# Attention scores of the first batch as whole fp32 matmuls over 64 rows, with the activation table loaded early

## The chip, the cores and the metric

The kernel runs on one core of a Trainium2 chip. The metric is the device time of one execution in microseconds. Before the change it was 1102.54 us, the median of three runs (1102.28 to 1103.45 us). All data is fp32.

## The reference

Three layers follow each other on 4 batches x 448 positions = 1792 tokens of width 768:

```python
scores = scale * np.matmul(q, k.transpose(0, 1, 3, 2))     # q, k, v: (4, 12, 448, 64)
scores = cap * np.tanh(scores / cap)
attn = np.exp(scores - np.max(scores, axis=-1, keepdims=True))
attn = attn / (np.sum(attn, axis=-1, keepdims=True) + 1e-09)
x = np.matmul(attn, v)                                     # heads side by side: (1792, 768)
h = np.maximum(np.maximum(x @ w1, x @ w2), x @ w3) @ w_out # 768 -> 768 -> 768
g = h @ w_gate                                             # 768 -> 1536
out = (g * (1 / (1 + np.exp(-g))) * (h @ w_val)) @ w_out2  # 1536 -> 768
```

## The kernel before

**Batches and units.** The dense layers of a batch are 60 units (`UNITS`); a unit is 18 float32r matmuls of 448 columns (L340) against one 128 x 768 block of weights. TensorE runs the units of batch 0, 1, 2, 3 in order. The attention of batch t+1 is spread over the units of batch t: for each of its 6 pairs of heads (`PAIRS`) the tables `SCORE_AT`, `WEIGH_AT`, `VALUE_AT`, `PREP_AT` name the unit that each part stands ahead of. Pair 6 is the first pair of batch 1, and its first scores, `scores(24)`, stand ahead of unit 0 in TensorE's program.

**The first batch's attention** has no dense work beside it. It is a phase of its own, of `FIRST` = 24 steps, four for each pair. A step `a` covers 2 x 112 keys: TensorE makes the scores (`scores`, L265, four float32r matmuls) into `score_ps` or, for odd steps, into two banks of `moe_ps`; ScalarE applies tanh (L395) and exp (L398) into `prob`; TensorE multiplies by v (`values_whole`, L279, two whole fp32 calls, four records). Half of the columns of `v_one` are ones, so that the same matmuls give the softmax sums. After a pair ScalarE copies the sums out (`take_sums`, L405), and VectorE takes the reciprocal (L502), multiplies (L505) and splits the result into `x_hi` and `x_lo` (`split_x`, L514 and L463). TensorE's order is scores(0), scores(1), then scores(a+2), values_whole(a) for each a; scores(a) waits for the tanh of step a-2. In this phase ScalarE also rounds the weights of the first four units (`weights_hi`, L386), one for each of the pairs 1 to 4.

**q and k.** `load_qk(g)` brings a pair's q and k, both heads, twice: into partitions 0 to 63 and again into 64 to 127 of one of the two halves of `qk_raw`. `prepare_qk(g, h)` on VectorE casts one head to `qk_hi` (L470), makes `q_lo` (L463) and subtracts in place for k (L463). The scores matmul thus has 128 rows: k high on the lower 64 and k low on the upper 64, against q in both.

**Queues.** Each engine works through its program in the order written. SyncE issues all loads in order: the qk and v loads of the first batch, then, unit by unit, `load_qk`, `load_v`, `store_lo` and `load_stage`; each has a wait ahead of it, and what stands behind waits with it. VectorE's order in the first phase is `prepare_qk(g + 1, 0)`, `normalise(g - 1)`, `split_x(0, g - 1)`, `prepare_qk(g + 1, 1)` for each g, and last `normalise(5)`, `split_x(0, 5)`. TensorE's units 0 to 2 leave the last chunk of x (pair 5) to the end of unit 2.

Of the kernel before, what the change touches and what calls it, by code (L numbers as in the profile page):

```python
# [9 lines left out]
ACT = mybir.ActivationFunctionType  # L10
ALU = mybir.AluOpType

P = 128
BATCH, HEADS, SEQ, HEAD_DIM = 4, 12, 448, 64
# [3 lines left out]
PAIRS = HEADS // 2  # L18
KEYS = 112
CH = SEQ // KEYS  # L20
HALF = CH // 2
# [13 lines left out]
JOBS = 54  # L35
NP = 4
NQ = 3

FIRST = 4 * PAIRS  # L40
# [31 lines left out]
def build(nc, w_in, qk_in, v_in, cap_in, out):  # L72
    ctx = ExitStack()
    with ctx:
        def sb(name, shape, dt=F32):
            return ctx.enter_context(nc.sbuf_tensor(name, shape, dt))
# [20 lines left out]
        qk_raw = sb("qk_raw", [P, 2, 4, SEQ])  # L97
# [10 lines left out]
        cap = sb("cap", [P, 1])  # L108
        inv_cap = sb("inv_cap", [P, 1])
        tanh_scale = sb("tanh_scale", [P, 1])  # L110

        moe_ps = ctx.enter_context(nc.psum_tensor("moe_ps", [P, BANKS, 512], F32))
        score_ps = ctx.enter_context(nc.psum_tensor("score_ps", [P, HALF, 512], F32))
# [47 lines left out]
        def score_banks(a):  # L161
            return moe_ps[:, 0:HALF, :] if a < FIRST and a % 2 else score_ps

        def value_banks(g):
            return moe_ps[:, 2:4, :] if g < PAIRS and g % 2 == 0 else pv_ps
# [3 lines left out]
        @block.sync  # L169
        def _(sp):  # L170
            def load_stage(u):
                if u >= UNITS + STAGE:
                    sp.wait_ge(w_hi_done, u - STAGE + 1)
                elif u >= STAGE:
                    sp.wait_ge(w_lo_done, u - STAGE + 1)
                sp.dma_start(stage[:, u % STAGE, :],
                             w_in[u % UNITS, :, :]).then_inc(w_loaded[u % STAGE], 16)

            def store_lo(u):
                sp.wait_ge(w_lo_done, u + 1)  # L180
                sp.dma_start(lo_store[u, :, :],
                             w_lo[:, u % R_LO, :].bitcast(F32)).then_inc(lo_stored[u % R_LO], 16)

            def load_lo(u):
                k = u % UNITS
                sp.wait_ge(unit_done, u - R_LO + 1)
                if u < UNITS + R_LO:
                    sp.wait_ge(lo_stored[u % R_LO], 16 * (UNITS // R_LO))
                sp.dma_start(w_lo[:, u % R_LO, :].bitcast(F32),  # L189
                             lo_store[k, :, :]).then_inc(lo_loaded[u % R_LO], 16)  # L190

            def load_qk(g):
                if g >= 2:
                    sp.wait_ge(qk_split, 2 * (g - 1))
                for r in range(2):
                    sp.dma_start(qk_raw[r * HEAD_DIM:(r + 1) * HEAD_DIM, g % 2, :, :],
                                 qk_in[g, :, :, :]).then_inc(qk_loaded[g % 2], 16)

            def load_v(g):
                if g < 2:  # L200
                    sp.wait_ge(ones_done, 4)
                elif g < PAIRS + 2:
                    sp.wait_ge(value_done, 4 * (g - 1))
                else:
                    sp.wait_ge(v_split, g - 1 - PAIRS)
                for h in range(2):
                    sp.dma_start(v_one[:, g % 2, h, :, v_cols[h]],
                                 v_in[g, :, h, :, :]).then_inc(v_loaded[g % 2], 16)

            sp.dma_start(cap[:, :], cap_in).then_inc(cap_loaded, 16)  # L210
            load_qk(0)
            load_v(0)
            load_qk(1)
            load_v(1)
            for u in range(STAGE):
                load_stage(u)
            for g in range(PAIRS):
                load_qk(g + 2)
                if g + 2 <= PAIRS:
                    load_v(g + 2)  # L220
            for u in range(LAST):
                t, k = divmod(u, UNITS)
                g, j = pair_of(t, k)
                if g is not None and j == 0 and PAIRS + 2 <= g + 2 < BATCH * PAIRS:
                    load_qk(g + 2)
                if g is not None and j == 2 and g + 1 < BATCH * PAIRS:
                    load_v(g + 1)
                if t == 0:
                    store_lo(u)
                if u + STAGE < LAST:  # L230
                    load_stage(u + STAGE)
                if UNITS <= u + R_LO < LAST:
                    load_lo(u + R_LO)
# [18 lines left out]

        @block.tensor
        def _(pe):
            def scores(a):
                g, h, c = a // 4, a // 2 % 2, a % 2
                pe.wait_ge(qk_split, 2 * g + h + 1)
                if a >= FIRST:
                    pe.wait_ge(tanh_done, a)
                elif a >= 2:  # L260
                    pe.wait_ge(tanh_done, a - 1)
                for i in range(HALF):
                    k0 = (HALF * c + i) * KEYS
                    for n, q in enumerate((qk_hi[:, h, :], q_lo[:, h, :])):
                        last = nc.tensor.matmul(score_banks(a)[0:KEYS, i, 0:SEQ],  # L265
                                                qk_hi[:, 2 + h, k0:k0 + KEYS], q,
                                                start=(n == 0), stop=(n == 1))
                last.then_inc(score_done, 1)

            def values_whole(a):  # L270
                g, h, c = a // 4, a // 2 % 2, a % 2
                if h == 0 and c == 0:
                    pe.wait_ge(v_loaded[g % 2], 32 * (g // 2 + 1))
                    if g >= 2:
                        pe.wait_ge(norm_done, g - 1)
                pe.wait_ge(exp_done, a + 1)
                for i in range(HALF):
                    j = HALF * c + i
                    last = nc.tensor.matmul(value_banks(g)[:, h, 0:SEQ], v_one[:, g % 2, h, j, :],  # L279
                                            prob[:, a % NP, i, :], start=(j == 0), stop=(j == CH - 1))  # L280
                last.then_inc(value_done, 1)

            def values_split(a):
# [71 lines left out]
                    bank_free(u)  # L355

            pe.wait_ge(ones_done, 8)
            scores(0)
            scores(1)
            for a in range(FIRST):  # L360
                if a + 2 < FIRST:
                    scores(a + 2)
                values_whole(a)
            for u in range(LAST):
                t, k = divmod(u, UNITS)
# [15 lines left out]
        def _(act):  # L381
# [17 lines left out]
                                     scale=cap[0:KEYS, 0:1]).then_inc(exp_done, 1)  # L399

            def take_sums(g, h):
                act.wait_ge(value_done, 4 * g + 2 * h + 2)
                if g >= 1:
                    act.wait_ge(inv_done, g)
                nc.scalar.activation(sums[v_cols[h], :], value_banks(g)[sum_cols[h], h, 0:SEQ],  # L405
                                     ACT.Copy).then_inc(sums_done, 1)

            def evacuate(u):
# [17 lines left out]
                elif k >= U_OUT2 and k % 2 == 1:  # L426
# [6 lines left out]
                    act.wait_ge(out_done, n + 1)  # L433
                    act.dma_start(out[b, :, t, :], out_sb[:, n % 2, :]).then_inc(stored[n % 2], 16)

            act.wait_ge(scale_done, 2)
            act.wait_ge(cap_loaded, 16)
            for a in range(FIRST):
                weigh(a)
                if a >= 2 and a % 2 == 1:  # L440
                    take_sums((a - 2) // 4, (a - 2) // 2 % 2)
                if a % 4 == 2 and 1 <= a // 4 <= R_HI:
                    weights_hi(a // 4 - 1)
            take_sums(PAIRS - 1, 1)
            for u in range(LAST):
                t, k = divmod(u, UNITS)
                g, j = pair_of(t, k)
# [13 lines left out]
        def _(dve):  # L461
# [3 lines left out]
            def prepare_qk(g, h):  # L465
                raw = qk_raw[:, g % 2, :, :]
                dve.wait_ge(qk_loaded[g % 2], 32 * (g // 2 + 1))
                if g >= 1:
                    dve.wait_ge(score_done, 4 * (g - 1) + 2 * h + 2)
                nc.vector.tensor_copy(qk_hi[:, h::2, :], raw[:, h::2, :]).then_inc(qk_hi_done, 1)  # L470
                dve.wait_ge(qk_hi_done, 2 * g + h + 1)
                subtract(q_lo[:, h, :], raw[:, h, :], qk_hi[:, h, :])
                subtract(qk_hi[low, 2 + h, :], raw[low, 2 + h, :],
                         qk_hi[low, 2 + h, :]).then_inc(qk_split, 1)
# [43 lines left out]
            def evacuate(u):  # L518
# [22 lines left out]
                elif k < U_OUT2:  # L541
# [6 lines left out]
                    else:  # L548
# [11 lines left out]
            dve.wait_ge(scale_done, 1)  # L560
            nc.vector.tensor_scalar(tanh_scale[:, :], inv_cap[:, :], HEAD_DIM ** -0.5, None,
                                    ALU.mult).then_inc(scale_done, 1)
            for h in range(2):
                prepare_qk(0, h)
            for g in range(PAIRS):
                prepare_qk(g + 1, 0)
                if g >= 1:
                    normalise(g - 1)
                    split_x(0, g - 1)
                prepare_qk(g + 1, 1)  # L570
            normalise(PAIRS - 1)
            split_x(0, PAIRS - 1)
            for u in range(LAST):
                t, k = divmod(u, UNITS)
                g, j = pair_of(t, k)
# [50 lines left out]
```

## Time and profile before

| | |
|---|---|
| median of the runs | 1102.54 us |
| the profiled execution | 1104.76 us, of which the span from first to last instruction is 1102.8 us |
| TensorE matmul busy | 1085.2 us (98%), 5232 matmuls |
| TensorE weight load busy | 980.7 us (89%) |
| VectorE busy | 582.6 us (53%) |
| ScalarE busy | 475.2 us (43%) |
| GpSimd busy | 121.1 us (11%) |
| HBM traffic | 201 GB/s over the span |

The busy shares are averages over a start of some 10 us, the attention phase of the first batch up to about 72 us, and the rest. Matmul records overlap each other (the end of one is modelled), so the distance from start to start is what a matmul costs, and the busy time is not. Every time of the timeline counts from the start of the span.

### The profile page before, as it was taken

What the parts mean: (1) busy time and instruction counts of PE and PEld (TensorE: products, weight loads), DVE (VectorE), ACT (ScalarE), POOL (GpSimd) and SP (SyncE); (2) the same over time, 40 slices, a digit from 0 to 9 for tenths busy, and PEclk for the clock granted to TensorE, in tenths of its full rate; (3) what the DMA queues carried; (4) which work ended last, traced back from release to release, by engine and by line L of the source; (5) the groups of instructions that cost most, each with busy time, mean ns of one, the idle gap of its engine ahead of it and who ended that gap; (6) DMA issues with size and microseconds to landing.
All of it is one profiled execution on the core that took longest, in us unless ns stands there. A gap on an engine that the chain in (4) does not pass through costs nothing.

```text
span 1102.8 us, 13696 instructions
## 1 busy us (share of the span) xinstructions
PE 1085.2 (98%) x5232; PEld 980.7 (89%) x5232; DVE 582.6 (53%) x794; ACT 475.2 (43%) x601; POOL 121.1 (11%) x72
## 2 busy tenths in 40 slices
PE   6999999999999999999999999999999999999998
PEld 3669999999998999999999999999999999999998
DVE  3998777988961555557553354555664212122310
ACT  5965444444433353454452434434443322332322
POOL 0105444444340000000000000000000000000000
PEclk9999999999999999999999999999999999999999
DMA  7566763754848577577476856765555766666664
GB/s 182 121 162 219 261 211 125 265 194 144 267 148 265 180 214 210 175 213 216 171 221 224 252 177 208 220 188 197 182 172 183 234 232 208 225 210 219 218 227 134
DMA packets 98897, 222.68 MB, mean 202 GB/s; under 512 B 31249, under 2 KB 34321, under 8 KB 98833
## 3 DMA queue, kind: packets, MB, share of 16 engines
q1 hardware_dynamic: 95376, 216.31, 62.1%
q10 hardware_dynamic: 3456, 5.51, 1.3%
q8 instruction: 42, 0.69, 0.3%
q14 instruction: 23, 0.18, 0.1%
HBM read 192.68 MB, written 29.10 MB: 201 GB/s over the span
## 4 chain that ended last, share of the span: by engine, by line
PE 92%; ACT 3%; issue 2%; DMA 2%; SPq 0%; DVE 0%; ACTq 0%
PE moe_ps L340 78%; PE score_ps L265 6%; PE pv_ps L292 5%; PE pv_ps L297 3%; ACT prob L395 2%; DMA lo_store<-w_lo 1%; DMA qk_raw<-qk_in 1%; ACT sums L405 0%; DMA stage<-w_in 0%; ACT w_hi L386 0%; PE moe_ps L279 0%; ACT prob L398 0%; PE pv_ps L279 0%; ACT L395 0%; SPq L189 0%
## 5 line engine op out<-in xcount | busy, mean ns | idle before, releaser
L340 PE MATMUL moe_ps<-x_lo,w_hi 128*128 128x448 f32 x1008 | 369.1, 366 | 0.0
L340 PE MATMUL moe_ps<-x_hi,w_hi 128*128 128x448 f32 x1008 | 368.9, 366 | 0.0
L340 PE MATMUL moe_ps<-x_hi,w_lo 128*128 128x448 f32 x1008 | 368.5, 366 | 0.0
L386 ACT ACTIVATE w_hi<-stage 128x768 fp32r<-128x768 f32 x240 | 202.3, 843 | 341.6 <-DMA stage<-w_in 212.0
L340 PEld LDWEIGHTS moe_ps<-x_hi,w_hi 128*128 128x128 f32 x1008 | 189.7, 188 | 16.1
L340 PEld LDWEIGHTS moe_ps<-x_hi,w_lo 128*128 128x128 f32 x1008 | 189.9, 188 | 15.1
L340 PEld LDWEIGHTS moe_ps<-x_lo,w_hi 128*128 128x128 f32 x1008 | 189.9, 188 | 15.0
L340 PE MATMUL moe_ps<-gv_hi,w_hi 128*128 128x448 f32 x432 | 157.9, 365 | 0.0
L340 PE MATMUL moe_ps<-gv_lo,w_hi 128*128 128x448 f32 x432 | 157.9, 365 | 0.0
L340 PE MATMUL moe_ps<-gv_hi,w_lo 128*128 128x448 f32 x432 | 157.7, 365 | 0.0
L249 POOL TENSOR_TENSOR w_lo<-stage,w_hi 128x768 fp32r<-128x768 f32 x60 | 118.9, 1983 | 208.4 <-ACT w_hi L386 208.4
L398 ACT ACTIVATE prob<-prob,cap 112x896 f32<-112x896 f32 x96 | 100.3, 1045 | 3.1
L463 DVE TENSOR_TENSOR p_lo<-prob,p_hi 112x896 fp32r<-112x896 f32 x72 | 93.9, 1305 | 2.5
L502 DVE RECIPROCAL inv<-sums 128x448 f32<-128x448 f32 x24 | 70.8, 2952 | 32.0 <-ACT sums L405 31.7
L340 PEld LDWEIGHTS moe_ps<-gv_hi,w_hi 128*128 128x128 f32 x432 | 81.1, 188 | 7.1 <-DVE gv_lo L463 0.4
L395 ACT ACTIVATE prob<-score_ps,tanh_scale 112x896 f32<-112x896 f32 x84 | 84.1, 1002 | 6.5 <-PE score_ps L265 6.0
L340 PEld LDWEIGHTS moe_ps<-gv_lo,w_hi 128*128 128x128 f32 x432 | 81.2, 188 | 6.4
L340 PEld LDWEIGHTS moe_ps<-gv_hi,w_lo 128*128 128x128 f32 x432 | 81.2, 188 | 6.4
L495 DVE CAST p_hi<-prob 112x896 fp32r<-112x896 f32 x72 | 44.7, 620 | 74.9 <-ACT prob L398 74.7
L265 PE MATMUL score_ps<-qk_hi 128*112 128x448 f32 x168 | 65.7, 391 | 14.4 <-DVE qk_hi L463 10.9
L425 ACT ACTIVATE sig<-moe_ps 128x448 f32<-128x448 f32 x48 | 26.1, 544 | 107.7 <-PE moe_ps L340 107.7
L528 DVE TENSOR_TENSOR work<-moe_ps,work 128x448 f32<-128x448 f32 x24 | 15.0, 624 | 105.7 <-PE moe_ps L340 105.6
(50 smaller groups left out, 893.0 us busy)
## 6 DMA issues: line engine op xcount, KB each, us to landing
stage<-w_in SPq DMA_DIRECT2D x240, 384.0 KB, 4.0
w_lo<-lo_store SPq DMA_DIRECT2D x180, 384.0 KB, 3.1
lo_store<-w_lo SPq DMA_DIRECT2D x60, 384.0 KB, 3.9
qk_raw<-qk_in SPq DMA_DIRECT2D x48, 448.0 KB, 6.2
v_one<-v_in SPq DMA_DIRECT2D x48, 112.0 KB, 3.8
out<-out_sb ACTq DMA_DIRECT2D x24, 224.0 KB, 4.4
cap<-cap_in SPq DMA_DIRECT2D x1, 0.5 KB, 2.0
```

Source lines behind the costliest of these rows:

```text
L249: nc.gpsimd.tensor_tensor(w_lo[:, s, :], stage[:, u % STAGE, :], w_hi[:, u % R_HI, :].bitcast(F32), ALU.subtract).then_inc(w_lo_done, 1)
L265: last = nc.tensor.matmul(score_banks(a)[0:KEYS, i, 0:SEQ], qk_hi[:, 2 + h, k0:k0 + KEYS], q, start=(n == 0), stop=(n == 1))
L292: nc.tensor.matmul(pv_ps[:, h, 0:SEQ], v[:, h, j, :], p_hi[:, a % NQ, i, :], start=(j == 0 and v is v_hi), stop=False)
L297: last = nc.tensor.matmul(pv_ps[:, h, 0:SEQ], v_hi[:, h, j, :], p_lo[:, a % NQ, i, :], start=False, stop=(j == CH - 1))
L340: mm = nc.tensor.matmul(moe_ps[:, bank_of(u), 0:SEQ], w[:, u % ring, c * P:(c + 1) * P], m[:, kc, :], start=(first and c == 0 and n == 0), ...
L386: nc.scalar.activation(w_hi[:, u % R_HI, :], stage[:, u % STAGE, :], ACT.Copy).then_inc(w_hi_done, 1)
L395: nc.scalar.activation(prob[:, a % NP, :, :], score_banks(a)[0:KEYS, :, 0:SEQ], ACT.Tanh, scale=tanh_scale[0:KEYS, 0:1]).then_inc(tanh_don ...
L398: nc.scalar.activation(prob[:, a % NP, :, :], prob[:, a % NP, :, :], ACT.Exp, scale=cap[0:KEYS, 0:1]).then_inc(exp_done, 1)
L425: nc.scalar.activation(sig[:, n % 2, :], ps, ACT.Tanh, scale=0.5).then_inc(gate_tanh, 1)
L463: return nc.vector.tensor_tensor(dst, whole, hi.bitcast(F32), ALU.subtract)
L495: nc.vector.tensor_copy(p_hi[:, a % NQ, :, :], prob[:, a % NP, :, :]).then_inc(p_hi_done, 1)
L502: nc.vector.reciprocal(inv[:, :], sums[:, :]).then_inc(inv_done, 1)
```

## The change

The scores of the first batch are no longer made from split operands. `load_qk(g)` for the pairs 0 to 5 brings head 0's q and k into partitions 0 to 63 and head 1's into 64 to 127, half of the bytes, with the wait ahead of it on `score_done` in place of `qk_split`. A step now covers 112 keys of both heads: `scores_whole(a)` is two whole fp32 calls, one on the rows 0 to 63 (head 0) and one on the rows 64 to 127 (head 1), each into a bank of its own. `values_whole(a)` multiplies both heads' `prob` of those keys, still two whole calls. `take_sums` of both heads come together, at the second step of the next pair. `prepare_qk` of the pairs 0 to 5 is gone; that of pair 6 stands behind `split_x(0, 5)` in VectorE's program. ScalarE does a tanh on one column (`table_warm`) as soon as `cap` is there, ahead of the first real one.

```diff
             def load_qk(g):
-                if g >= 2:
-                    sp.wait_ge(qk_split, 2 * (g - 1))
+                if 2 <= g < PAIRS + 2:
+                    sp.wait_ge(score_done, 4 * (g - 1))
+                elif g >= PAIRS + 2:
+                    sp.wait_ge(qk_split, 2 * (g - 1 - PAIRS))
                 for r in range(2):
-                    sp.dma_start(qk_raw[r * HEAD_DIM:(r + 1) * HEAD_DIM, g % 2, :, :],
-                                 qk_in[g, :, :, :]).then_inc(qk_loaded[g % 2], 16)
+                    rows = slice(r * HEAD_DIM, (r + 1) * HEAD_DIM)
+                    if g < PAIRS:
+                        sp.dma_start(qk_raw[rows, g % 2, 0:2, :],
+                                     qk_in[g, :, r::2, :]).then_inc(qk_loaded[g % 2], 16)
+                    else:
+                        sp.dma_start(qk_raw[rows, g % 2, :, :],
+                                     qk_in[g, :, :, :]).then_inc(qk_loaded[g % 2], 16)
...
+            def scores_whole(a):
+                g, c = a // 4, a % 4
+                pe.wait_ge(qk_loaded[g % 2], 32 * (g // 2 + 1))
+                if a >= 2:
+                    pe.wait_ge(tanh_done, a - 1)
+                for h in range(2):
+                    rows = slice(h * HEAD_DIM, (h + 1) * HEAD_DIM)
+                    last = nc.tensor.matmul(score_banks(a)[0:KEYS, h, 0:SEQ],
+                                            qk_raw[rows, g % 2, 1, c * KEYS:(c + 1) * KEYS],
+                                            qk_raw[rows, g % 2, 0, :], start=True, stop=True)
+                last.then_inc(score_done, 1)
+
             def scores(a):
                 g, h, c = a // 4, a // 2 % 2, a % 2
-                pe.wait_ge(qk_split, 2 * g + h + 1)
-                if a >= FIRST:
-                    pe.wait_ge(tanh_done, a)
-                elif a >= 2:
-                    pe.wait_ge(tanh_done, a - 1)
+                pe.wait_ge(qk_split, 2 * (g - PAIRS) + h + 1)
+                pe.wait_ge(tanh_done, a)
...
             def values_whole(a):
-                g, h, c = a // 4, a // 2 % 2, a % 2
-                if h == 0 and c == 0:
+                g, c = a // 4, a % 4
+                if c == 0:
...
-                for i in range(HALF):
-                    j = HALF * c + i
-                    last = nc.tensor.matmul(value_banks(g)[:, h, 0:SEQ], v_one[:, g % 2, h, j, :],
-                                            prob[:, a % NP, i, :], start=(j == 0), stop=(j == CH - 1))
+                for h in range(2):
+                    last = nc.tensor.matmul(value_banks(g)[:, h, 0:SEQ], v_one[:, g % 2, h, c, :],
+                                            prob[:, a % NP, h, :], start=(c == 0), stop=(c == CH - 1))
...
+            act.wait_ge(cap_loaded, 16)
+            nc.scalar.activation(table_warm[:, :], cap[:, :], ACT.Tanh)
             act.wait_ge(scale_done, 2)
-            act.wait_ge(cap_loaded, 16)
             for a in range(FIRST):
                 weigh(a)
-                if a >= 2 and a % 2 == 1:
-                    take_sums((a - 2) // 4, (a - 2) // 2 % 2)
+                if a % 4 == 1 and a > 4:
+                    for h in range(2):
+                        take_sums(a // 4 - 1, h)
...
-            take_sums(PAIRS - 1, 1)
+            for h in range(2):
+                take_sums(PAIRS - 1, h)
...
+            for g in range(PAIRS):
+                normalise(g)
+                split_x(0, g)
             for h in range(2):
-                prepare_qk(0, h)
-            for g in range(PAIRS):
-                prepare_qk(g + 1, 0)
-                if g >= 1:
-                    normalise(g - 1)
-                    split_x(0, g - 1)
-                prepare_qk(g + 1, 1)
-            normalise(PAIRS - 1)
-            split_x(0, PAIRS - 1)
+                prepare_qk(PAIRS, h)
```

## Rows read from the trace of the kernel before

**Rows 1.** the page, part 4: shares of the chain that ended last, by line
```profile
PE moe_ps L340 78%; PE score_ps L265 6%; PE pv_ps L292 5%; PE pv_ps L297 3%; ACT prob L395 2%; DMA lo_store<-w_lo 1%; DMA qk_raw<-qk_in 1%; ACT sums L405 0%; DMA stage<-w_in 0%; ACT w_hi L386 0%; PE moe_ps L279 0%; ACT prob L398 0%; PE pv_ps L279 0%; ACT L395 0%; SPq L189 0%
```

**Rows 2.** chain of waits, first 16 us: start, length, engine, tile, line
```profile
1.79 5.79 DMA qk_raw<-qk_in
...
9.67 1.82 PE score_ps L265 x4
11.59 1.28 ACT L395
12.88 1.02 ACT prob L395
...
14.03 1.81 PE score_ps L265 x4
```

**Rows 3.** the page, part 6: issues, count, KB each, median us to landing
```profile
qk_raw<-qk_in SPq DMA_DIRECT2D x48, 448.0 KB, 6.2
...
cap<-cap_in SPq DMA_DIRECT2D x1, 0.5 KB, 2.0
```

**Rows 4.** timeline, TensorE, one step: start us, busy us, engine, line, operation, tiles
```profile
22.48 0.71 PE L265 MATMUL moe_ps<-qk_hi 128*112 128x448 f32 x1
...
23.02 0.37 PE L265 MATMUL moe_ps<-q_lo,qk_hi 128*112 128x448 f32 x1
...
23.23 0.36 PE L265 MATMUL moe_ps<-qk_hi 128*112 128x448 f32 x1
...
24.79 0.71 PE L265 MATMUL score_ps<-qk_hi 128*112 128x448 f32 x1
```

**Rows 5.** timeline, TensorE, the values' four matmuls early and later
```profile
15.63 2.72 PE L279 MATMUL moe_ps<-prob,v_one 112*128 112x448 f32 x4
...
17.84 0.71 PE L265 MATMUL moe_ps<-qk_hi 128*112 128x448 f32 x1
...
19.00 1.67 PE L279 MATMUL moe_ps<-prob,v_one 112*128 112x448 f32 x4
```

**Rows 6.** timeline, ScalarE, one pair of heads
```profile
35.99 0.54 ACT L405 ACTIVATE sums<-pv_ps 64x448 f32<-64x448 f32 x1
...
36.55 1.01 ACT L395 ACTIVATE prob<-score_ps,tanh_scale 112x896 f32<-112x896 f32 x1
...
37.59 1.04 ACT L398 ACTIVATE prob<-prob,cap 112x896 f32<-112x896 f32 x1
...
38.54 0.83 ACT L386 ACTIVATE w_hi<-stage 128x768 fp32r<-128x768 f32 x1
...
46.57 1.01 ACT L395 ACTIVATE prob<-score_ps,tanh_scale 112x896 f32<-112x896 f32 x1
```

**Rows 7.** timeline, all engines, 66 to 74 us
```profile
66.62 2.95 DVE L502 RECIPROCAL inv<-sums 128x448 f32<-128x448 f32 x1 [0.63 <-ACT sums L405]
...
70.72 1.77 PE L279 MATMUL pv_ps<-prob,v_one 112*128 112x448 f32 x4 [0.20 <-ACT prob L398]
...
71.87 0.62 DVE L470 CAST qk_hi<-qk_raw 128x896 fp32r<-128x896 f32 x1
...
71.98 0.71 PE L265 MATMUL score_ps<-qk_hi 128*112 128x448 f32 x1
...
72.53 0.54 ACT L405 ACTIVATE sums<-pv_ps 64x448 f32<-64x448 f32 x1 [1.29 <-PE pv_ps L279]
...
73.14 0.36 PE L340 MATMUL moe_ps<-x_hi,w_hi 128*128 128x448 f32 x1
...
73.17 0.62 DVE L463 TENSOR_TENSOR qk_hi<-qk_raw,qk_hi 64x448 fp32r<-64x448 f32 x1
```

**Rows 8.** timeline, SyncE's own queue, same stretch
```profile
64.52 10.40 SPq L196 DMA_DIRECT2D qk_raw<-qk_in  x4
```

**Rows 9.** waits of TensorE after 73 us: total us, times, longest us
```profile
PE score_ps L265 <- ACT prob L395: 2.4, 1, 2.4
```

**Rows 10.** windows: us, PE PEld DVE ACT POOL busy (x), clock, DMA, GB/s
```profile
348.00:353.00 5.00, 5.00 (x19) 4.51 (x18) 1.72 (x2) 1.06 (x2) 0.00 (x0) 0.66 0.96 207
```

More of the change, by code:

```diff
@@ L110, in build @@
         tanh_scale = sb("tanh_scale", [P, 1])
+        table_warm = sb("table_warm", [P, 1])
         moe_ps = ctx.enter_context(nc.psum_tensor("moe_ps", [P, BANKS, 512], F32))
@@ L357, in _ @@
             pe.wait_ge(ones_done, 8)
-            scores(0)
-            scores(1)
+            scores_whole(0)
+            scores_whole(1)
             for a in range(FIRST):
                 if a + 2 < FIRST:
-                    scores(a + 2)
+                    scores_whole(a + 2)
                 values_whole(a)
@@ L401, in take_sums @@
             def take_sums(g, h):
-                act.wait_ge(value_done, 4 * g + 2 * h + 2)
+                act.wait_ge(value_done, 4 * g + (4 if g < PAIRS else 2 * h + 2))
                 if g >= 1:
@@ L467, in prepare_qk @@
                 dve.wait_ge(qk_loaded[g % 2], 32 * (g // 2 + 1))
-                if g >= 1:
+                if g > PAIRS:
                     dve.wait_ge(score_done, 4 * (g - 1) + 2 * h + 2)
                 nc.vector.tensor_copy(qk_hi[:, h::2, :], raw[:, h::2, :]).then_inc(qk_hi_done, 1)
-                dve.wait_ge(qk_hi_done, 2 * g + h + 1)
+                dve.wait_ge(qk_hi_done, 2 * (g - PAIRS) + h + 1)
                 subtract(q_lo[:, h, :], raw[:, h, :], qk_hi[:, h, :])
@@ L562, in _ @@
                                     ALU.mult).then_inc(scale_done, 1)
+            for g in range(PAIRS):
+                normalise(g)
+                split_x(0, g)
             for h in range(2):
-                prepare_qk(0, h)
-            for g in range(PAIRS):
-                prepare_qk(g + 1, 0)
-                if g >= 1:
-                    normalise(g - 1)
-                    split_x(0, g - 1)
-                prepare_qk(g + 1, 1)
-            normalise(PAIRS - 1)
-            split_x(0, PAIRS - 1)
+                prepare_qk(PAIRS, h)
             for u in range(LAST):
```

## The prediction

> **What bounds the kernel now.** I read the chain of waits first. By line it belongs to TensorE's unit matmuls (L340) for 78% of the span [rows 1], and TensorE's own waits from 73 us to the end hold only one of note, 2.4 us [rows 9]. So after 73 us nothing but TensorE's order counts, and what the change does before that point moves the end by the same amount, one for one. The question is when the first unit's first matmul starts; now that is at 73.14 us [rows 7].
>
> Before that point three stretches differ. At the start the chain goes through the load of q and k (landed at 1.79 + 5.79 = 7.6), VectorE's splitting (to 9.67), the first scores, and then 1.28 us on ScalarE before its first tanh at 12.88 [rows 2]; that piece is the table load. In the middle, ScalarE is the bound: a pair's tanh starts at 36.55 and its counterpart one pair on at 46.57, 10.02 us or 2.50 us a step [rows 6]. The work accounts for it: 4 x (1.04 from tanh to exp, plus 0.95 from exp to the next), two sums of 0.54, and 0.83 for a weight block [rows 6], together 9.9 us. TensorE has a natural pace of 2.31 us a step (22.48 to 24.79) [rows 4], just below that. At the end of the phase there is no gap at all: values(23) starts at 70.72 and scores(24), for which pair 6 is long split, follows in TensorE's queue at 71.98 [rows 7].
>
> **Unit costs.** A float32r matmul costs 0.20 us from start to start (23.02 to 23.23) [rows 4]. A step has four of them, 0.81 us, so the values' four records take the other 1.50 us, 0.375 each: a whole fp32 call is two records, 0.75 us.
>
> **Part 1, the start.** The split leaves the chain. The load is halved: both issues (448 KB each) took 5.79 us from the second issue on [rows 2], while 0.5 KB takes 2.0 us [rows 3]. I take 2.0 fixed and half of the other 3.8: landing at 1.79 + 3.9 = 5.7, first scores at 5.8 instead of 9.67. The bounds are 3.9 (a load as quick as the small one) and 7.7 (no gain, since the pieces are shorter). The table load goes under the wait for this load: `cap` is there some 2 us after its issue [rows 3], long before any score.
>
> **Part 2, the step on TensorE.** The values stay at 1.50 us. The scores were 0.81 us for 4 x 0.20; now they are two whole calls on different halves of the rows, four records of 0.375. No row shows matmuls on parts of the array. The bounds are 0.75 us (the two calls entirely at once) and 1.50 us (one after the other). I choose between: the records come in the order A1, A2, B1, B2, A2 has to wait for A1 since both use the rows 0 to 63, and B1 can start beside A2 but not ahead of it. That gives three times 0.375, 1.12 us. Each step also changes twice between halves of the array and the whole. The nearest row is the change from float32r to whole matmuls, which costs nothing (2.31 = 0.81 + 1.50). The other end is an array that must empty: values(23)'s records occupy 4 x 0.375 = 1.50 us and ScalarE sees them done after 72.53 - 70.72 = 1.81 [rows 7], so emptying takes about 0.3 us less the semaphore; I bound a change at 0.27 and take 0.05, near the row that shows nothing. Step: 1.12 + 1.50 + 0.10 = 2.72 us, 10.9 a pair. That is more than ScalarE's 10.02, so TensorE becomes the bound of the phase; 24 steps are 65.3 us.
>
> What the rows bear out here is only the price of a record. The Trainium skill, "TensorE: Matmul & The Clock Gate", Part 3, says that matmuls on different row groups overlap, their starts some 4 ns apart, though in strict order. With full overlap the sum would be that of rival A; read with the strict order, it is my 1.12 us. No trace shows either.
>
> **Part 3, the array's clock.** The values' records at 15.63 take 2.72 us for four, those at 19.00 take 1.67 [rows 5]; from 9.67 to 17.84 [rows 2, 5] TensorE works at half rate after its idle start, with one pause: the first scores take 1.82 us, the second 4 x 0.375 = 1.5, to 13.0, and the third start at 14.03 [rows 2]. That is 7.1 us of work at half rate, 3.5 us lost. (The granted clock reads 1.00 there; the durations say otherwise.) The other row is the one late gap: TensorE idles 2.4 us [rows 9], and of 348 to 353 us the mean granted clock is 0.66 [rows 10], a mixture of the levels 2.4 and 1.2 GHz, which costs 5 x 0.34 = 1.7 us. I take 2.6 us for a start after long idleness, bounds 1.7 and 3.5. At the kernel's start this is paid now and stays inside the phase.
>
> So values(23) is seen done at 5.8 + 65.3 + 2.6 + 0.3 = 74.0 us, against 72.53 now: after an earlier start of 3.9 us the phase ends 1.5 us later.
>
> **Part 4, the end of the phase.** This is the largest term. `prepare_qk(6, 0)` was done before pair 5's sums existed. Now it stands in VectorE's order behind `normalise(5)` and `split_x(0, 5)`, which wait for both sums, which wait for values(23). scores(24) waits for it, and behind scores(24) in TensorE's order stands every unit; nothing else can go ahead. The length from the rows: two sums of 0.54 (the first is now here too) 1.1 us, 0.05 to the reciprocal, from the reciprocal's start to the cast of the next pair 71.87 - 66.62 = 5.25, cast and two subtractions 73.17 + 0.62 - 71.87 = 1.92 [rows 7], and 0.14 from the last subtraction to the first scores [rows 2]: 8.5 us with TensorE idle. scores(24) starts at 82.5 and the first unit matmul 0.9 us later, at 83.4, against 73.14: 10.3 us later. TensorE has then idled for 8.5 us, longer than the 2.4 us that cost the clock before, so 2.6 us more go at the start of the units. Sum: +12.9 us.
>
> **Edits that I cost at nothing.** `load_qk(2)` to `load_qk(5)` wait for a pair's last scores in place of an early split. Behind them in SyncE's queue stands `load_v`. The landing takes 6.2 us at 448 KB [rows 3] and the scores that need it are four steps, 10.9 us, after the wait is met; were it later, its excess would come once for each of four pairs. `load_qk(8)`, behind which unit 4's weights queue, already waits now for pair 6's split: its issue stretches over 10.40 us from 64.52 [rows 8]. It stays as far behind scores(24) as it is. The sums of one pair taken together lengthen one ScalarE step by 0.54 and shorten another; ScalarE has 0.9 us a pair to spare.
>
> The profiled execution took 1104.76 us with a span of 1102.8, 2.2 us above the median of the runs. The sum is a difference, so I put it on the median: 1102.5 + 12.9 = 1115.4 us.
>
> **Rivals.**
> A, full overlap of the two heads: the step is 0.75 + 1.50 + 0.10 = 2.35 us, under ScalarE's 2.50, and ScalarE stays the bound. Its first tanh comes 1.9 us after the first scores begin (9.67 to 11.59 for as many half-rate record times), at 7.7 rather than 12.88, 5.2 us gained; the end of the phase costs 8.7 and the clock 2.6 us. Sum +6.1, 1108.6 us; 1106.7 with the quickest load. For it: the operands and banks are disjoint. Against: the order of the records.
> B, no overlap at all, the change doesn't do what it says on the array: 24 x 0.38 = 9.1 us above the forecast without switching (2.4 less), 1122 to 1124.5 us. For it: no row shows two matmuls at once.
> C, each change of division empties the array: 48 changes at 0.27 in place of 0.05 add 10.6 us, 1126 us. Against: nothing of the kind appears between kinds of matmul. The Trainium skill, "TensorEngine Tiling (Array Packing)", Key Properties, has this rule: a change of tiling mode drains TensorE. It speaks against the change, and no row here can show it.
> D, the other side: the gap late in the run [rows 9] closes because the queues meet differently, which returns 2.4 + 1.7 = 4.1 us, on top of A. The losses at the end of the phase, 8.7 + 1.7 at least, then outweigh it unless the first tanh starts 6.3 us earlier, before 6.6 us. With the quickest load it would start at 5.8: 1101.7 us. It needs three things at once.
>
> **How the numbers follow.** Forecast 0.45, A 0.18, B 0.20, C 0.12, D 0.02, and 0.03 for A with part of D, which ends within 0.2%. About 0.2% (2.2 us) is what a measurement of this kernel can tell from no change. Slower: 0.45 + 0.18 + 0.20 + 0.12 = 0.95, same 0.03, faster 0.02. The range goes from 1107 (A) to 1126 (B whole, C up to its centre); it leaves out D and half of C, and holds the forecast's own bounds: load 1.9 us and clock 1.8 us to either side, switching 2.4 us down.
>
> **What the profile after would show.** Scores starting near 5.8 us and the table load before them (part 1). A step of 2.7 us, with ScalarE waiting for scores; 2.5 us with ScalarE full would be A, 3.0 B, 3.2 C. In the chain at the end of the phase, sums, reciprocal, split of x, then L470 and L463 of pair 6, TensorE idle 8.5 us, and a granted clock under 1.00 behind it. The prediction is wrong if TensorE doesn't idle there, or if the step isn't near 2.7 us.

## The result and the profile after

The changed kernel takes 1110.41 us (median of four runs, 1110.01 to 1111.43) against 1102.41 us before: 8.0 us more, a ratio of 1.0072 with a 95% interval of 1.0055 to 1.0090. It is slower, as forecast, by less than the 12.9 us of the prediction, inside its range.

The profiled execution took 1110.43 us with a span of 1108.5 us. From the page: span, busy times, and the chain's share by engine (before, 92% of the chain lay on TensorE and 3% on ScalarE).

```profile
span 1108.5 us, 13649 instructions
...
PE 1090.0 (98%) x5232; PEld 967.8 (87%) x5232; DVE 562.0 (51%) x758; ACT 475.1 (43%) x602; POOL 121.0 (11%) x72
...
PE 97%; DMA 2%; DVE 1%; SPq 0%; issue 0%; ACT 0%; ACTq 0%
```

The chain of waits of the changed kernel up to the first units (start, length, engine, tile, line, number of records). L271 is the new scores line, L296 the values, L283 and L490/L483 the scores and the split of later pairs, L357 the units.

```profile
1.88 3.63 DMA qk_raw<-qk_in
...
5.64 1.83 PE score_ps L271 x4
7.48 1.49 PE moe_ps L271 x4
8.97 1.47 PE score_ps L271 x4
...
25.34 0.94 PE score_ps L271 x4
26.28 1.70 PE pv_ps L296 x4
27.98 0.94 PE moe_ps L271 x4
...
65.88 4.72 PE pv_ps L296 x12
...
71.76 2.96 DVE inv L522
...
77.09 0.55 DVE qk_hi L490
...
77.66 0.62 DVE q_lo L483
...
78.30 0.63 DVE qk_hi L483
...
78.98 1.84 PE score_ps L283 x4
80.81 3.62 PE moe_ps L357 x15
84.43 0.81 PE score_ps L283 x4
```

The first scores start at 5.64 us, where they started at 9.67 [rows 2]. Then TensorE alone carries the chain to 70.6 us: a step is 0.94 + 1.70 = 2.64 us, and from about 12 us on every step is alike. Before, ScalarE set the pace with 10.02 us a pair [rows 6]; now it is 10.56 us, and ScalarE waits for scores:

```profile
18.41 1.01 ACT L412 ACTIVATE prob<-moe_ps,tanh_scale 112x896 f32<-112x896 f32 x1 [0.56 <-PE moe_ps L271]
```

(timeline, ScalarE). values(23) is seen done at 70.63 us, 1.9 us earlier than before [rows 7]. That is the gain of the start and not of the step: the first scores come 4.0 us earlier, while the phase from there on takes 65.0 us in place of 62.8, since a step's scores now cost TensorE 1.14 us (2.64 - 1.50) where the split ones cost 0.81. Behind values(23) TensorE stands still. TensorE's waits of the whole run (total us, times, longest):

```profile
PE score_ps L283 <- DVE qk_hi L483: 8.4, 1, 8.4
PE score_ps L271 <- DMA qk_raw<-qk_in: 5.6, 1, 5.6
PE score_ps L283 <- ACT prob L412: 1.5, 1, 1.5
```

The first of these lines is new: scores(24) waits for pair 6's split, and the chain shows what the split waits for, the sums, the reciprocal and the split of x of pair 5. The third answers rows 9, a gap late in the run, 2.4 us before. The granted clock, in windows of one microsecond (us; busy of PE, PEld, DVE, ACT, POOL with instructions; clock; DMA share; GB/s):

```profile
75.00:76.00 1.00, 0.00 (x0) 0.00 (x0) 0.99 (x2) 0.00 (x0) 0.00 (x0) 0.52 0.00 0
...
80.00:81.00 1.00, 1.00 (x5) 0.84 (x4) 0.95 (x3) 0.15 (x1) 0.00 (x0) 0.50 0.00 0
...
82.00:83.00 1.00, 1.00 (x6) 0.92 (x5) 0.10 (x2) 0.94 (x1) 0.00 (x0) 1.00 0.95 222
```

TensorE has been idle since 70.6 us, the clock is at its lower level, 1.2 GHz, from about 75, stays there when work begins at 78.98, and is back at 2.4 GHz from about 81.9. The scores of step 25 start at 84.43 us, against 76.34 us in the chain before:

```profile
72.49 0.81 PE score_ps L265 x4
...
76.34 0.81 PE score_ps L265 x4
```

These are 8.1 us, about what the medians differ by: 1.9 us gained at the phase's end, 8.35 us of idling, and 1.6 us in the scores and units behind it (84.43 - 78.98 = 5.45 us, 3.85 before). The two profiled spans differ by 5.7 us only, because before's profiled execution lost 0.9 us more in the late gap and 1.7 us to the low clock behind it [rows 9, 10], some 2.6 us together. The part on the sum, below, comes back to that.

### The profile page after: what moved, and what is told of

It is laid out like the page before. It is cut to its first block, busy times and chain, and to the rows that moved or that the text cites. A ratio compares the mean times of both kernels' runs of the same rounds, so it can differ in the third digit from the quotient of the medians.

```text
span 1108.5 us, 13649 instructions
## 1 busy us (share of the span) xinstructions
PE 1090.0 (98%) x5232; PEld 967.8 (87%) x5232; DVE 562.0 (51%) x758; ACT 475.1 (43%) x602; POOL 121.0 (11%) x72
## 4 chain that ended last, share of the span: by engine, by line
PE 97%; DMA 2%; DVE 1%; SPq 0%; issue 0%; ACT 0%; ACTq 0%
PE moe_ps L357 78%; PE score_ps L283 5%; PE pv_ps L309 5%; PE pv_ps L314 3%; PE moe_ps L296 2%; PE pv_ps L296 2%; PE score_ps L271 1%; PE moe_ps L271 1%; DMA lo_store<-w_lo 1%; DMA stage<-w_in 0%; DMA qk_raw<-qk_in 0%; DVE inv L522 0%; DVE x_next L525 0%; ACT prob L412 0%; SPq L191 0%
## 5 line engine op out<-in xcount | busy, mean ns | idle before, releaser
L357 PE MATMUL moe_ps<-x_lo,w_hi 128*128 128x448 f32 x1008 | 368.7, 366 | 0.0
L357 PE MATMUL moe_ps<-x_hi,w_hi 128*128 128x448 f32 x1008 | 368.6, 366 | 0.0
L357 PE MATMUL moe_ps<-x_hi,w_lo 128*128 128x448 f32 x1008 | 368.0, 365 | 0.0
L357 PEld LDWEIGHTS moe_ps<-x_hi,w_hi 128*128 128x128 f32 x1008 | 189.6, 188 | 16.2
L357 PEld LDWEIGHTS moe_ps<-x_lo,w_hi 128*128 128x128 f32 x1008 | 189.6, 188 | 15.0
L357 PEld LDWEIGHTS moe_ps<-x_hi,w_lo 128*128 128x128 f32 x1008 | 189.5, 188 | 15.0
L357 PE MATMUL moe_ps<-gv_hi,w_hi 128*128 128x448 f32 x432 | 157.9, 366 | 0.0
L357 PE MATMUL moe_ps<-gv_lo,w_hi 128*128 128x448 f32 x432 | 157.9, 365 | 0.0
L357 PE MATMUL moe_ps<-gv_hi,w_lo 128*128 128x448 f32 x432 | 157.7, 365 | 0.0
L483 DVE TENSOR_TENSOR p_lo<-prob,p_hi 112x896 fp32r<-112x896 f32 x72 | 95.5, 1326 | 2.5
L357 PEld LDWEIGHTS moe_ps<-gv_hi,w_hi 128*128 128x128 f32 x432 | 81.1, 188 | 7.1 <-DVE gv_lo L483 0.4
L357 PEld LDWEIGHTS moe_ps<-gv_lo,w_hi 128*128 128x128 f32 x432 | 81.2, 188 | 6.4
L357 PEld LDWEIGHTS moe_ps<-gv_hi,w_lo 128*128 128x128 f32 x432 | 81.1, 188 | 6.4
L566 DVE SCALAR_TENSOR_TENSOR sig<-sig,moe_ps 128x448 f32<-128x448 f32 x48 | 29.8, 621 | 76.5 <-ACT sig L442 76.3
```

Source lines behind the costliest of these rows:

```text
L357: mm = nc.tensor.matmul(moe_ps[:, bank_of(u), 0:SEQ], w[:, u % ring, c * P:(c + 1) * P], m[:, kc, :], start=(first and c == 0 and n == 0), ...
L483: return nc.vector.tensor_tensor(dst, whole, hi.bitcast(F32), ALU.subtract)
```

## The experiments

### Taking the wait away: split_early, early4, filler

In VectorE's order of the changed kernel, pair 6's split goes to another place:

```diff
             for g in range(PAIRS):
+                if g == PAIRS - 1:
+                    for h in range(2):
+                        prepare_qk(PAIRS, h)
                 normalise(g)
                 split_x(0, g)
-            for h in range(2):
-                prepare_qk(PAIRS, h)
```

> The changed kernel with one edit: VectorE splits q and k of pair 6 ahead of normalise(5) and not behind split_x(0, 5). Theory (the time is lost in the wait of scores(24) for this split): TensorE's idle of 8.4 us (70.6 to 78.98 us) goes, and with it the half clock behind it (1.4 us); the first unit matmul comes at 71 to 72 us in place of 80.61, and the median falls from 1110.4 to about 1100.7 us, below the kernel before. Rival 1 (the loss is in the phase's matmuls): no change, 1110.4 us. Rival 2 (another wait stands right behind: the sums of pair 5, or the first units' weights): half or less of the 8.4 us comes back, 1105 us or more.

Measured: 1101.57 us, ratio to the kernel before 0.9991 (0.9982 to 1.0000). 8.8 us come back with one edit, so rival 1 falls. TensorE still waited 0.5 us for the split, which stood behind the normalising of pair 4. `early4` has `PAIRS - 2` in place of `PAIRS - 1`:

> The changed kernel with pair 6's split ahead of normalise(4) in VectorE's order, one place earlier than in the last such run. There the split still ended 0.7 us after TensorE was free (71.36 us against 70.6), since it stood behind normalise(4). Theory: the rest of the wait goes, scores(24) follows values(23) at 70.4 to 70.7 us, and the median is 0.7 us below the last one's 1101.6: 1100.9. Rival (the sums of pair 4, which now wait behind the split, hold up TensorE or the first units' banks): no gain or a loss, 1101.6 us or more.

Measured: 1100.56 us, ratio 0.9984 (0.9975 to 0.9993): 9.85 us less than the changed kernel. The terms read from the changed kernel's trace give 8.35 us of idling and 1.6 us behind it, 9.95 together. The chain of early4 has no gap any more:

```profile
65.47 4.71 PE pv_ps L296 x12
70.17 0.81 PE score_ps L283 x4
70.98 3.09 PE moe_ps L357 x15
```

The clock's part was measured by itself, by filling the wait and leaving it as long as it is:

```diff
+            pe.wait_ge(w_hi_done, 1)
+            pe.wait_ge(x_ready, 1)
+            for i in range(38):
+                nc.tensor.matmul(score_ps[:, 0, 0:SEQ], w_hi[:, 0, 0:P], x_hi[:, 0, :],
+                                 start=True, stop=True)
             for u in range(LAST):
```

> The changed kernel with 38 float32r matmuls of 448 columns added between values(23) and scores(24), into a bank that scores(24) then overwrites; they read the first block of rounded weights and of x, and their product is thrown away. They take 38 x 0.20 = 7.7 us of the 8.4 us that TensorE waits there. Theory (the array's clock falls in the idle time and costs time behind it): the wait stays, scores(24) still starts near 79 us, but its four matmuls and the first unit's run at 0.20 us apiece, and 1.4 us come back, 1109.0 us. Rival (the half rate is no result of idling, or the matmuls add work): 1110.4 us or more.

Measured: 1109.15 us, 1.3 us less than the changed kernel, by doing 38 useless matmuls more. In the chain of filler the scores still start at 78.8 us, but run at full rate (1.07 against 1.84 us, 3.09 against 3.62):

```profile
78.80 1.07 PE score_ps L283 x4
79.87 3.09 PE moe_ps L357 x15
```

So 1.3 of the 1.6 us behind the idling are the clock's. The other 0.3 remain in filler (4.15 us from scores to scores, 3.85 before), and scores(24) takes 1.07 us too behind the wait of 0.5 us in split_early, where the clock had not fallen; what they are made of wasn't tested.

### What a step is made of: all_rows, same_rows, upper_rows, one_half

The prediction had put the two heads' scores at 1.12 us, overlapped by half, and a change between half of the array and the whole at 0.05. The trace after gives 0.94 + 1.70. The sum of the two readings is nearly the same, so the step alone can't tell them apart. Four kernels could; each changes `rows` in `scores_whole` alone:

```diff
-                    rows = slice(h * HEAD_DIM, (h + 1) * HEAD_DIM)
+                    rows = slice(0, HEAD_DIM)                      # same_rows
+                    rows = slice(0, P)                             # all_rows
+                    rows = slice(HEAD_DIM, P)                      # upper_rows
+                    rows = slice(0, HEAD_DIM) if h == 0 else slice(0, P)   # one_half
```

> The changed kernel with both calls of a step over all 128 rows; the scores of both heads are thereby summed, and the output isn't the reference's. No call is on a part of the array. Theory 1 (a change of division costs 0.19 us): without any change 1.50 + 1.50 = 3.00 us a step, 0.38 less than with both calls on the rows 0 to 63. Theory 2 (changes are free): 3.00 too, the same as there, within 0.02.

> The changed kernel with both calls of a step on the rows 0 to 63; head 1's scores are replaced by head 0's, so that part of the output is head 0's weights on head 1's v. The phase's step is 2.64 us now. Theory 1 (the two heads overlap entirely, 0.75 us, and each change between halves of the array and the whole costs 0.19 us): the overlap goes and the two changes stay, 1.50 + 1.50 + 2 x 0.19 = 3.38 us a step, 24 x 0.74 = 17.8 us more. Theory 2, that of the prediction (the calls overlap by half, 1.12 us, and a change costs next to nothing, 0.01): 1.50 + 1.50 + 0.02 = 3.02 us, 9.1 us more. Theory 3 (no overlap now): no change.

Measured: all_rows 1119.69 us, and same_rows 1161.85 us, the latter far above either theory. Two chains, one after the other; first all_rows:

```profile
35.20 1.50 PE score_ps L271 x4
36.71 1.50 PE moe_ps L296 x4
38.21 1.50 PE moe_ps L271 x4
```

then same_rows, in the middle and near the end of the phase:

```profile
70.67 3.26 PE moe_ps L271 x4
73.92 3.27 PE moe_ps L296 x4
77.19 1.68 PE score_ps L271 x4
78.88 1.70 PE moe_ps L296 x4
80.58 1.68 PE moe_ps L271 x4
```

In same_rows every piece up to 77 us takes twice what it takes afterwards: the array was at half rate for the first 71 us of its work, which costs some 35 us and hides what was asked. The pieces behind 77.19 answer it: 1.68 + 1.70 = 3.38 us a step (3.39 from start to start), as theory 1 has it. With all 128 rows in both calls the step is 3.01 us from start to start (35.20 to 38.21), so 0.38 us depend on the calls being on half of the rows. If the two changes cost that, it is 0.19 each; if each half call cost it by itself, one_half, which has one half call and both changes, would show half of it.

> The changed kernel with head 0's call on the rows 0 to 63 as it is and head 1's call over all 128 rows, so that head 1's scores are those of both heads summed and the output isn't the reference's. Nothing can overlap, and a step has two changes between half and whole, as the changed kernel has. Theory 1 (full overlap in the changed kernel and 0.19 us for a change): 1.50 + 1.50 + 0.38 = 3.38 us a step. Theory 2 (changes nearly free, overlap by half): 3.02 us. If the array stays at half rate for a while, as it did with both calls on the rows 0 to 63, the steps after it rises are the ones to read.

Measured: 1133.34 us. Its chain once the rate is full:

```profile
24.87 1.50 PE moe_ps L296 x4
26.37 1.87 PE moe_ps L271 x4
28.24 1.50 PE moe_ps L296 x4
```

1.87 + 1.50 = 3.37 us. Both changes are there (the half call, then the whole one), and nothing overlaps. That is theory 1 again, 3.38, against 3.02, and the whole 0.37 is there with one half call: the price belongs to the change. So a step of the changed kernel is 0.75 for both heads' scores at once, 1.50 for the values, and 2 x 0.195 for the changes. The overlap is also plain in the changed kernel's own start: the scores of step 1 there, at half rate and with no change beside them, take 1.49 us, which is four records of 0.745 two at a time; overlapped by half they would take 2.24. And the timeline of the changed kernel shows the records starting two at a time at full rate (x2), with nothing between 14.71 and 15.18. Each pair must be one record of either call, since two on the same rows don't overlap (same_rows):

```profile
14.71 0.63 PE L271 MATMUL score_ps<-qk_raw 64*112 64x448 f32 x2
...
15.18 0.54 PE L271 MATMUL score_ps<-qk_raw 64*112 64x448 f32 x2
```

> The changed kernel with both calls of a step on the rows 64 to 127, where the earlier run had both on 0 to 63; the output isn't the reference's, since head 0 gets head 1's scores. That run stayed at half rate from its first matmul at 5.8 us to 77 us, without idling, and then went on at 3.38 us a step. Theory (the array at work on half of its rows for half of the time is what keeps the clock low, whichever half it is): the same here, half rate for 50 us or more, some 1160 us. Rival (a chance of that one execution, or something of the lower rows): full rate within 10 us, 1110.4 + 17.8 = 1128 us. Either way the step at full rate is 3.38 us.

Measured: 1146.0 us. Again the rate was half at first, here up to 44.5 us; the chain of upper_rows around it:

```profile
41.28 3.18 PE pv_ps L296 x4
44.47 1.68 PE moe_ps L271 x4
46.15 1.70 PE pv_ps L296 x4
```

The step behind it is 3.38 us once more, and the long spell at half rate is no feature of the lower rows. Its length, 71 us and 39 us in one execution of each, isn't explained by these runs; the expected 50 us or more was off for this one.

### Fewer changes: early4_two

If a change costs 0.19 us, two steps' scores followed by two steps' values save half of them:

```diff
-            for a in range(FIRST):
-                if a + 2 < FIRST:
-                    scores_whole(a + 2)
-                values_whole(a)
+            for a in range(0, FIRST, 2):
+                for i in range(2):
+                    if a + 2 + i < FIRST:
+                        scores_whole(a + 2 + i)
+                for i in range(2):
+                    values_whole(a + i)
```

> The same with TensorE's order changed: the scores of two steps, then the values of two steps, so that there is one change to half rows and one back for two steps. Theory 1 (a change costs 0.19 us): two steps take 2 x 2.25 + 2 x 0.19 = 4.88 us in place of 5.28; that is 2.44 a step, just under ScalarE's 2.50, so ScalarE is the bound and the phase gets 24 x 0.14 = 3.4 us shorter: 1097.5 us. Theory 2 (changes nearly free, overlap by half, which adjacent scores would extend to 1.88 for four calls): 4.88 too. Rival (the engines wait for each other in pairs of steps): a step stays at 2.64 or grows, 1100.9 us or more.

Measured: 1096.94 us, ratio 0.9951 (0.9936 to 0.9966), faster than both kernels. Its chain:

```profile
20.20 0.94 PE score_ps L271 x4
21.14 0.75 PE moe_ps L271 x4
21.89 3.21 PE pv_ps L296 x8
25.10 0.94 PE score_ps L271 x4
...
67.27 0.82 PE score_ps L283 x4
```

The first scores after the values cost 0.94, the next 0.75: the 0.19 belongs to the change and not to the scores. Two steps take 4.90 us (25.10 - 20.20), where 4.88 was expected. TensorE's order has 21 changes in place of 43, and 22 fewer at 0.195 us are 4.3 us. The phase, from the first scores to scores(24), got 2.7 us shorter (61.6 against 64.35 us), because early4's execution came to full rate sooner. Its spell at half rate lasted 3.0 us, that of early4_two 5.9: scores(2) take 0.87 us in the one chain and 1.60 in the other. The medians differ by 3.6 us; early4's profiled execution was 0.8 us faster than its median. TensorE remains in the chain, so ScalarE's pace of 2.50 us a step, which the expectation took for a floor, is not one: in this kernel a pair takes 9.8 us, and ScalarE waits for scores once only, 0.7 us.

### The start: full_load, no_table, before_table, roused

full_load gives the first batch the loads of the kernel before, and reads the same q and k from them:

```diff
-                    if g < PAIRS:
-                        sp.dma_start(qk_raw[rows, g % 2, 0:2, :],
-                                     qk_in[g, :, r::2, :]).then_inc(qk_loaded[g % 2], 16)
...
-                                            qk_raw[rows, g % 2, 1, c * KEYS:(c + 1) * KEYS],
-                                            qk_raw[rows, g % 2, 0, :], start=True, stop=True)
+                                            qk_raw[rows, g % 2, 2 + h, c * KEYS:(c + 1) * KEYS],
+                                            qk_raw[rows, g % 2, h, :], start=True, stop=True)
```

> The changed kernel with q and k of the pairs 0 to 5 loaded whole into both halves of the partitions, as the kernel before does (448 KB a load in place of 224); the scores read the same values. Theory (the halved load brings the first scores forward by what it is shorter, since nothing else is on the path): the first scores start 2.0 us later, at 7.6 to 7.8 in place of 5.64 us, and the whole run takes 2.0 us more, 1112.4 us. Rival (the extra bytes cost nothing at the end, since the later start is taken up by the array's low clock or by ScalarE's lead): 1110.4 to 1111 us.

Measured: 1113.23 us, 2.8 us more than the changed kernel. The first scores start at 7.84 us, 2.2 us later, and values(23) is seen done at 73.06, 2.4 us later; 0.2 of that are a longer spell at half rate. The halved load is worth at least what was claimed for it.

no_table takes the early tanh out:

```diff
-            nc.scalar.activation(table_warm[:, :], cap[:, :], ACT.Tanh)
```

> The changed kernel without the tanh on one column, so that the table is loaded when the first scores are there. Theory: scores(2) waits for the first tanh and values(0) for the first exp, so all of TensorE's steps move by the 1.28 us of the load: 1111.7 us. Rival (TensorE is the bound of the phase and has a lead): 0.3 us or less, 1110.7 us.

Measured: 1113.63 us, 3.2 us more and not 1.3. The chain of no_table at the start:

```profile
7.70 1.28 ACT L412
...
10.14 1.84 PE score_ps L271 x4
11.98 2.48 PE moe_ps L296 x4
```

Here TensorE waits 1.1 us for the first tanh, and then does scores(2) wholly and values(0) mostly at half rate (1.84 and 2.48 us; 1.47 and 1.70 in the changed kernel). values(23) is seen done 2.3 us later: 1.1 for the wait, 1.1 to 1.2 for the slower pieces, 0.1 for a later landing. The remaining 0.9 us lie behind the phase; 0.4 of them are again a longer spell (the first unit's piece is 4.04 us, 3.62 in the changed kernel).

before_table is the kernel before with this one line added (and the column it writes):

> The kernel before with one part of the change alone: the tanh on one column as soon as cap is there. Theory (ScalarE bounds the first phase there, and its first tanh waits for the table load after the first scores): the first tanh starts at 11.6 us in place of 12.88 and all that follows moves with it, 1.3 us less, 1101.2 us. Rival (TensorE's or VectorE's work takes over, since the later steps have little slack): 0 to 0.6 us less, 1102 to 1102.5 us.

Measured: 1100.98 us, ratio 0.9987 (0.9977 to 0.9997), 1.5 us less than the kernel before. The scores that follow values(23) start at 71.06 us in its chain, against 72.49 before. So 1.4 us are gained where they were expected, and this part of the change is a gain by itself.

roused adds to early4_two five throw-away matmuls under the wait for the first load:

```diff
+            pe.wait_ge(ones_done, 1)
+            for i in range(5):
+                nc.tensor.matmul(score_ps[0:HEAD_DIM, 0, 0:CH * HEAD_DIM], v_one[:, 0, 0, 0, sum_cols[0]],
+                                 v_one[:, 0, 0, :, sum_cols[0]], start=True, stop=True)
             pe.wait_ge(ones_done, 8)
```

> The fastest version so far (pair 6 split ahead of normalise(4), scores and values of two steps together, 1096.9 us) with five small whole matmuls of ones by ones ahead of scores(0), while TensorE waits for the load; their product is thrown away. They start near 1.1 us and take some 5 x 0.85 = 4.3 us at half rate, to 5.4 us, just ahead of the load. Theory (what the array did before sets how long it stays at half rate): it rises to full rate earlier than now (near 10.7 us), and of the some 2.3 us lost there 1 to 2 us come back: 1095.0 to 1096.0 us. Rival (small matmuls of ones don't rouse it): 1096.9 us; rival 2 (they run past the load): up to 1 us more.

Measured: 1096.63 us, ratio 0.9951 (0.9934 to 0.9967). The timeline of roused (TensorE) shows that the small matmuls do what they are there for, and that the gain doesn't follow:

```profile
1.10 4.26 PE L376 MATMUL score_ps<-v_one 112*64 112x256 f32 x10 [1.10 <-POOL v_one L248]
5.80 1.01 PE L271 MATMUL score_ps<-qk_raw 64*112 64x448 f32 x4 [0.43 <-DMA qk_raw<-qk_in]
...
10.03 1.01 PE L271 MATMUL moe_ps<-qk_raw 64*112 64x448 f32 x4 [0.96 <-ACT prob L418]
```

The scores run at full rate from the first one (1.01 against 1.84 us), but scores(2) and scores(3) then wait for ScalarE's tanh, 0.5 and 0.96 us. scores(24) starts 1.1 us earlier (66.20 against 67.27 in the chains), and of that 0.3 us is seen in the medians, whose spans overlap: no difference that these runs can tell. The expectation of 1 to 2 us was wrong because ScalarE's first two steps stand right behind TensorE's.

## Why the prediction was right, and where its steps were off

**The load (part 1)**: right. 5.8 us predicted for the first scores, 5.64 measured; full_load puts the term at 2.2 us of start and 2.8 us of time.

**The step (part 2)**: its size nearly right, 2.72 predicted and 2.64 measured, its composition wrong. The argument from the order of the records failed (A1, A2, B1, B2, with B1 beside A2): A1 starts with B1 and A2 with B2, so the two calls overlap entirely, 0.75 us and not 1.12. The price of a change was put near a row that has no such change, 0.05; it is 0.195 (all_rows against same_rows, one_half, and 0.94 against 0.75 in early4_two). The errors, 0.37 too much for the overlap and 2 x 0.145 too little for the changes, nearly cancel; that the step's size came out so near is luck. Rival A had the overlap right, rival C the existence of the cost, and the truth is both together: no rival combined them. TensorE took over as the bound as forecast; under rival A alone it would not have. The rule of the Trainium skill ("TensorE: Matmul & The Clock Gate", Part 3) that matmuls on different row groups overlap agrees with the trace: 0.75 us for both calls in early4_two. The Trainium skill also has the rule that a change of tiling mode drains the engine ("TensorEngine Tiling (Array Packing)", Key Properties), to which the prediction gave a chance of 0.12. That a change costs time agrees: 0.195 us at full rate, and 0.28 to 0.30 in same_rows at half rate (3.26 and 3.28 less 4 x 0.745). That the time is spent on draining is not shown here.

The prediction also counted 48 changes. TensorE's order has 43: the first three scores stand together, and the last three values. At the true price that is 1.0 us.

**The clock (part 3)**: the mechanism right, both sizes too large. At the start 2.6 us were put on it. The phase took 70.63 - 5.64 = 65.0 us; 24 x 2.25 for the matmuls, 43 x 0.195 for the changes and 0.3 until the end is seen make 62.7, and the other 2.3 are the clock's and a short wait's. Behind the idle time 2.6 us were predicted and 1.4 measured: half rate lasted 2.9 us from 78.98. filler is the direct measurement, 1.3 us.

**The end of the phase (part 4)**: right, to 0.15 us. TensorE idles 8.35 us where 8.5 was worked out from rows 7 and 2, and for the reason given. split_early and early4 show that it is the cause of the result: without it the change is 1.9 us faster than the kernel before.

**The sum.** 12.9 - 8.0 = 4.9 us too much, of which these terms make 4.75: values(23) done at 70.63 and not 74.0 (3.4, of which the step's size 1.9, the changes that aren't there 1.0, the rest the start and the clock), 0.15 in the wait, 1.2 in the clock behind it. The late gap of rival D is shorter in the changed kernel's trace, 1.5 us and without a fall of the clock. But before's profiled execution, in which the clock fell behind that gap, was 2.2 us above the median of its runs. So most executions of before probably lack the fall, and the medians don't owe their difference to it; that is argued, since only one of them has a trace.

**The edits costed at nothing** cost nothing: TensorE has no wait for a load of the pairs 1 to 5 in any of these traces, and its order behind scores(24) holds no wait for weights.

## What to carry to other kernels

Work that is taken out of an engine's order uncovers what was placed among it: pair 6's split was hidden between those of earlier pairs, and once these were gone it stood at the end, behind the one chain that TensorE waits for. Follow the first consumer of each moved piece. When matmuls on halves of the array are mixed with whole ones, count the changes, and put the halves next to each other: here that was worth 3.6 us. The overlap is worth 24 x 0.75 = 18 us against two calls one after the other, but with the changes the new scores are still dearer for TensorE than the split ones, 1.14 against 0.81 us a step. And a long wait can cost TensorE more than its length: that of 8.35 us cost 1.3 us more, since the clock was low when work resumed. Behind the gap of 1.5 us it didn't fall.

## What the runs showed of the hardware that I had not expected

Two whole fp32 calls of 64 rows each, on different halves of the array, take the time of one (0.75 us for 448 columns), though each is two records: the first records of both start together (14.71, x2), then the second ones (15.18, x2). A change between half and whole costs 0.195 us at the higher level of the clock.

After an idle start, TensorE's spell at half rate had very different lengths. In the changed kernel, both halves in use at once, it was 4.5 us (5.64 to about 10.2). Kernels whose TensorE starts with the same pieces were at it from 3.0 us (early4) to 5.1 us (full_load). So differences of up to 2 us aren't the edits' work, and what is put on this spell above, in no_table and full_load too, is what single traces show. With all rows it was 4.2 us (all_rows, 5.83 to about 10.0), and in roused 3.9 us, counted from the small matmuls. In one_half it was over 14 us. In same_rows and upper_rows, with the scores on one half only and values between them, it was 71 and 39 us without any idling. What decides that isn't settled by single executions, but a kernel that leaves half of its rows unused at the start may pay for it with tens of microseconds.

The granted clock reads 1.00 in the windows at the start of every trace, in same_rows for 71 us while all matmuls take double. The traces' own records of the clock begin with its first rise (at 10.19 us in the changed kernel, at 77.05 us in same_rows), so the 1.00 ahead of that is no measurement; from there on it agrees with the durations. The ends of the spells above are these first rises. At the start of an execution the rate has to be read from the matmuls. The same_rows window, with 14 records in 10 us:

```profile
60.00:70.00 10.00, 10.00 (x14) 3.41 (x12) 4.59 (x4) 5.67 (x7) 0.00 (x0) 1.00 0.10 23
```
